# Attention and two feed-forward stages on one core: unread matmuls in front of and among the early heads, and the splitting of x and of most weights moved between engines

## The reference

```python
B, H, S, D = 4, 8, 576, 64                      # batch, heads, positions, width of a head
scores = q @ k.T / sqrt(D);  scores[block_i < block_j] = -1e9      # blocks of 64 positions
attn = exp(scores - max) / (sum + 1e-9);  x = attn @ v             # x: 2304 tokens x 512
h = maximum(maximum(x @ w1, x @ w2), x @ w3)                       # 768 wide
y = h @ w_out                                                      # 512 wide
h2 = y @ w_in;  g = h2 * cos(h2);  out = g @ w_out2                # 2048 wide, back to 512
```

## Time and profile before

| | us |
|---|---|
| median of 3 runs (1001.79 to 1003.62) | 1003.39 |
| the profiled execution, its own time | 1003.43 |
| its span, first to last instruction | 1001.6 |
| PE busy | 967.4 (97%) |
| PEld busy | 874.0 (87%) |
| DVE busy | 579.4 (58%) |
| ACT busy | 572.1 (57%) |
| POOL busy | 188.6 (19%) |

### The profile page before, as it was taken

The page is one execution under the profiler, slowest core; times in us unless marked ns, Lnnn a source line. Parts: engine busy times, 40 slices in busy tenths (PEclk is TensorE's granted clock), DMA queues, the critical chain, the costliest instruction groups (busy, mean ns, idle before and its releaser), DMA issues.

```text
span 1001.6 us, 16447 instructions
## 1 busy us (share of the span) xinstructions
PE 967.4 (97%) x5808; PEld 874.0 (87%) x5808; DVE 579.4 (58%) x1155; ACT 572.1 (57%) x1294; POOL 188.6 (19%) x168
## 2 busy tenths in 40 slices
PE   7998899999999999999999999999999999999998
PEld 6877789889989989999999987789999999999996
DVE  5665566776455655555411257767657566576564
ACT  4576465676455555555322256676656666666665
POOL 2385312322221212212134412210000000000000
PEclk9997799999999999999999999999999999999999
DMA  9242222232222222121051060010010010100000
GB/s 259 60 123 56 61 83 77 79 89 76 71 60 72 60 61 72 49 71 38 19 187 56 1 211 13 1 64 1 1 64 0 0 63 0 63 0 0 31 1 32
DMA packets 58144, 58.16 MB, mean 58 GB/s; under 512 B 26048, under 2 KB 42208, under 8 KB 58080
## 3 DMA queue, kind: packets, MB, share of 16 engines
q1 hardware_dynamic: 55824, 56.73, 18.9%
q10 hardware_dynamic: 2256, 0.59, 0.3%
HBM read 47.78 MB, written 9.52 MB: 57 GB/s over the span
## 4 chain that ended last, share of the span: by engine, by line
PE 73%; DVE 7%; ACT 6%; issue 3%; POOL 1%; ACTq 0%
PE M_ps L670 8%; PE M_ps L672 7%; PE M_ps L671 7%; PE T_ps L625 6%; PE O_ps L643 5%; PE S_ps L743 3%; PE S_ps L536 3%; PE S_ps L742 3%; PE S_ps L741 3%; PE M_ps L680 3%; DVE rest L948 3%; PE M_ps L719 2%; PE O_ps L719 2%; PE M_ps L717 2%; PE O_ps L717 2%
## 5 line engine op out<-in xcount | busy, mean ns | idle before, releaser
L670 PE MATMUL M_ps<-x,w_h 128*128 128x288 f32 (+2 forms) x576 | 178.5, 310 | 0.9 <-POOL w_l L1237 0.9
L672 PE MATMUL M_ps<-x,w_h 128*128 128x288 f32 (+2 forms) x576 | 171.3, 297 | 0.0
L671 PE MATMUL M_ps<-x,w_l 128*128 128x288 f32 (+2 forms) x576 | 171.3, 297 | 0.0
L1185 ACT ACTIVATE away<-rest 128x384 f32<-128x384 f32 x96 | 50.4, 525 | 115.2 <-DVE rest L948 115.2
L670 PEld LDWEIGHTS M_ps<-x,w_h 128*128 128x128 f32 x576 | 109.8, 191 | 3.6 <-issue 1.0
L671 PEld LDWEIGHTS M_ps<-x,w_l 128*128 128x128 f32 x576 | 110.1, 191 | 0.0
L672 PEld LDWEIGHTS M_ps<-x,w_h 128*128 128x128 f32 x576 | 109.9, 191 | 0.0
L849 DVE TENSOR_TENSOR pt_l<-T_ps,pt_h 128x384 fp32r<-128x384 f32 (+2 forms) x120 | 68.9, 574 | 55.1 <-ACT pt_h L1107 55.0
L1091 ACT ACTIVATE prob<-S_ps,neg_max 128x512 f32<-128x512 f32 (+4 forms) x144 | 83.0, 582 | 16.9 <-DVE neg_max L834 16.9
L1107 ACT ACTIVATE pt_h<-T_ps 128x384 fp32r<-128x384 f32 (+2 forms) x120 | 60.6, 505 | 54.3 <-PE T_ps L625 50.7
L625 PE MATMUL T_ps<-ident,prob 128*128 128x128 f32 (+2 forms) x456 | 88.5, 282 | 0.0
(11 more groups left out here) (138 smaller groups left out, 2451.0 us busy)
## 6 DMA issues: line engine op xcount, KB each, us to landing
k_raw<-kT SPq DMA_DIRECT2D x64, 144.0 KB, 2.8
q_raw<-qT SPq DMA_DIRECT2D x48, 144.0 KB, 2.7
y_raw<-y_d SPq DMA_DIRECT2D x6, 768.0 KB, 4.6
out<-o_out SPq DMA_DIRECT2D x18, 256.0 KB, 2.1
v_raw<-v SPq DMA_DIRECT2D x32, 128.0 KB, 2.7
win_raw<-w_in SPq DMA_DIRECT2D x16, 256.0 KB, 6.5
w_raw<-w_out SPq DMA_DIRECT2D x16, 256.0 KB, 5.5
inv_b<-inv_d SPq DMA_DIRECT2D x24, 144.0 KB, 3.1
```

The lines of the kernel that those rows point to most:

```text
L670: mm(o, w_h, x_h, start=k == 0, stop=False)
L671: mm(o, w_l, x_h, start=False, stop=False)
L672: last = mm(o, w_h, x_l, start=False, stop=k == KM - 1)
```

## The change

PE starts with 12 matmuls of 512 columns on a tile of zeros (`WARM`), whose result nobody reads, and from the third early head on puts one more unread matmul of 512 columns in front of each head's scores. The mask of the early heads is added on the 64 rows of the head instead of on all 128. In the main part the high part of x is written by ACT; its low part stays on DVE but stands later in the period. All pieces of w1, w2, w3 and w_out are 512 elements wide; their low parts, and those of w_out2, are made by DVE. POOL keeps those of w_in. Pieces of the first feed-forward stage are split in periods 0 to 6 instead of 0 to 4, at places named W in the orders instead of at the end of the period. `piece`, `early` and `walk` follow this.

```diff
-LAG = {"tA": 1, "tB0": 1, "tB1": 1, "tB2": 1, "vA": 1, "vB": 1, "inv": 1, "inv_out": 1, "inv_in": 1, "take": 1, "norm": 2,
-       "split": -1, "load": -2, "load_v": -1}
+LAG = {"tA": 1, "tB0": 1, "tB1": 1, "tB2": 1, "vA": 1, "vB": 1, "inv": 1, "inv_out": 1, "inv_in": 1, "take": 1,
+       "norm": 2, "norm_low": 2, "split": -1, "load": -2, "load_v": -1}
...
-DVE_PERIOD = ["inv", "sA", "tA", "sC", "tB0", "norm", "G2", "tB1", "sD", "tB2", "split", "G1", "take", "G3"]
-ACT_PERIOD = ["tA", "eA", "tB0", "eC", "G2", "tB1", "split", "tB2", "eD", "G1", "take", "split_v", "G3"]
+DVE_PERIOD = ["inv", "sA", "tA", "sC", "tB0", "norm", "G2", "tB1", "sD", "tB2", "split", "norm_low", "G1", "W1", "take", "W2", "G3"]
+ACT_PERIOD = ["tA", "eA", "tB0", "eC", "G2", "tB1", "norm", "split", "W2", "tB2", "eD", "W1", "G1", "take", "split_v", "G3"]
...
-SP_PERIOD = ["load", "G2", "inv_out", "G1", "inv_in", "load_v", "G3"]
+SP_PERIOD = ["load", "G2", "inv_out", "G1", "inv_in", "load_v", "W1", "G3"]
...
-W_COLS = [(0, P), (P, P), (2 * P, 2 * P), (4 * P, 2 * P)]
-W_OF = [next(n for n, (c0, w) in enumerate(W_COLS) if c0 <= f * P < c0 + w) for f in range(KF1)]
-PIECES = [("w%d" % (j + 1), None, n) for n in range(len(W_COLS)) for j in range(3)]
+PIECES = [("w%d" % (j + 1), None, f * P) for f in range(KF1) for j in range(3)]
...
-PIECES += [("w_out", k, 0) for k in range(0, KF1, 2)]
+PIECES += [("w_out", k, 0) for k in range(KF1)]
...
-W_AHEAD = 12
...
+W_EARLY_HIGH = {4: (0,), 5: (1,), 6: (2,)}
+W_EARLY_LOW = {8: (0, 1), 9: (2,)}
+W_HIGH = {0: (3, 4, 5), 1: (6, 7, 8, 9), 2: (10, 11, 12), 3: (13, 14, 15), 4: (16, 17, 18), 5: (19, 20, 21), 6: (22, 23)}
+W_LOW = W_HIGH
...
+W_AHEAD = 18
...
-        if s[0] == "G":
-            out += ["G"] * ((slots + places - int(s[1:])) // places)
+        if s[0] in "GW":
+            places = sum(o[0] == s[0] for o in names)
+            out += [s[0]] * (((slots if s[0] == "G" else pieces) + places - int(s[1:])) // places)
...
+WARM = 12
...
+            if name == "W":
+                if pieces:
+                    step("weights", pieces.pop(0))
...
+        consts_set, warm_set = sem("consts_set"), sem("warm_set")
+        w_high, w_low, win_low, w2_low = sem("w_high"), sem("w_low"), sem("win_low"), sem("w2_low")
...
-                return (wo_raw[:, k:k + 2, :], wo_h[:, k:k + 2, :], wo_l[:, k:k + 2, :],
-                        w_out[k * P:(k + 2) * P, :].rearrange("(k p) f -> p k f", p=P))
+                return wo_raw[:, k, :], wo_h[:, k, :], wo_l[:, k, :], w_out[k * P:(k + 1) * P, :]
...
                     pe.wait_ge(e_exped, a - 3)
                 half, p = slice(D * (a % 2), D * (a % 2) + D), a // 2
+                if a >= 2:
+                    mm(E_ps[a % 4], mask_l[:], ke_h[:, 0:2, :].rearrange("p a s -> p (a s)"), start=True, stop=True)
                 for t in SCORES["A"]:
                     n, tile = KEYS[t], slice(P * t, P * (t + 1))
                     o = E_ps[a % 4][:, S_AT[t]:S_AT[t] + n]
                     mm(o, qe_h[half, p, tile], ke_h[half, p, 0:n], start=True, stop=False)
                     mm(o, qe_h[half, p, tile], ke_l[half, p, 0:n], start=False, stop=False)
                     mm(o, qe_l[half, p, tile], ke_h[half, p, 0:n], start=False, stop=False)
-                    last = mm(o[:, n - BLOCK:n], mask_l[:], mask_r[:], start=False, stop=True)
+                    last = mm(o[:, n - BLOCK:n], mask_l[half, :], mask_r[half, :], start=False, stop=True)
...
-                        pe.wait_ge(w_low, W_OF[f] * 3 + j + 1)
+                        pe.wait_ge(w_low, f * 3 + j + 1)
...
-                            if c == 0 and k % 2 == 0:
-                                pe.wait_ge(w_low, N_W123 + k // 2 + 1)
+                            if c == 0:
+                                pe.wait_ge(w_low, N_W123 + k + 1)
...
+
+            pe.wait_ge(warm_set, 1)
+            for _ in range(WARM):
+                mm(O_ps[:, 0:BANK], pt_l[:, 0:P], pt_l[:, 0:BANK], start=True, stop=True)
...
-                    pe.wait_ge(w_low, N_IN + f + 1)
+                    pe.wait_ge(w2_low, f + 1)
...
+            def split_weights(p):
+                raw, hi, lo, _ = piece(p)
+                dve.wait_ge(w_high, p + 1)
+                V.tensor_tensor(lo, raw, hi.bitcast(F32), ALU.subtract).then_inc(w_low if p < N_P1 else w2_low, 1)
...
                 V.tensor_tensor(mine, mine, inv_b[:, pair % 2, q0:], ALU.mult).then_inc(x_normed, 1)
-                dve.wait_ge(x_normed, pair + 1)
+
+            def normalise_low(n):
+                q0, b, pair = first_query(n), n // H, n // 2
+                mine = x_f[:, pair % 2, q0:]
                 hi, lo = (x[:, b % 2, part, pair % KM, q0:] for part in range(2))
-                V.tensor_scalar(hi, mine, 1.0, None, ALU.mult).then_inc(x_high, 1)
                 dve.wait_ge(x_high, pair + 1)
                 V.tensor_tensor(lo, mine, hi.bitcast(F32), ALU.subtract).then_inc(x_lowed, 1)
...
+            V.memset(pt_l[:, 0:BANK].bitcast(F32), 0.0).then_inc(warm_set, 1)
...
-            V.memset(mask_l[0:1, 0:BLOCK].bitcast(F32), 1.0).then_inc(consts_set, 1)
-            early(early_step, DVE_EARLY)
-            walk(step, DVE_PERIOD)
+            for row in (0, D):
+                last = V.memset(mask_l[row:row + 1, 0:BLOCK].bitcast(F32), 1.0)
+            last.then_inc(consts_set, 1)
+            early(early_step, DVE_EARLY, W_EARLY_LOW)
+            walk(step, DVE_PERIOD, W_LOW)
...
-            def chunk(c):
+            def chunk(c, split=False):
 
                 last = isinstance(c, int) and c == NC2 - 1
                 for f in range(1, KF2):
                     tile(c, f, last)
+                    if split:
+                        split_weights(N_IN + f)
...
-            chunk(0)
+            split_weights(N_IN)
+            chunk(0, split=True)
...
+            def normalise(n):
+                q0, b, pair = first_query(n), n // H, n // 2
+                act.wait_ge(x_normed, pair + 1)
+                A(x[:, b % 2, 0, pair % KM, q0:], x_f[:, pair % 2, q0:], ACT.Copy).then_inc(x_high, 1)
...
-            early(early_step, ACT_EARLY)
-            walk(step, ACT_PERIOD)
+            early(early_step, ACT_EARLY, W_EARLY_HIGH)
+            walk(step, ACT_PERIOD, W_HIGH)
...
-                sub(lo, raw, hi.bitcast(F32), ALU.subtract).then_inc(w_low, 1)
+                sub(lo, raw, hi.bitcast(F32), ALU.subtract).then_inc(win_low, 1)
...
-                elif name == "weights":
-                    split_weights(a)
...
-            for p in range(N_IN, len(PIECES)):
-                split_weights(p)
```

38 lines of the change are left out of this document (19 added, 19 removed).

## The result

The changed kernel takes 986.96 us (median of 4 runs, 985.13 to 988.22), the kernel before 1003.5 us beside it: ratio 0.9838, 95% interval 0.9818 to 0.9857. It is faster by 16.5 us (1.6%), not by 32.5, and lies outside the range. The profiled executions have spans of 985.7 and 1001.6 us, 15.9 us apart.

What follows compares the result with a forecast made beforehand. PE, with a matmul in flight 97% of the span, was taken as the bound; gains of 6 + 15 + 0.5 + 0.5 + 10.5 = 32.5 us off 1003.43 gave 971 us, own range 966 to 975, 8 times in 10 962 to 982.

Steps and rivals of the forecast that it cites:

- Nobody waits for x until the next batch's groups: Main part: the reason given why ACT can write x's high parts, eight more in each half; no cost set for it.
- the third stretch near 137 us: Main part: third stretch of lowered granted clock (0.71 over 135 to 140 us), left as it is, no gain counted.
- A: Early heads: at full clock DVE sets the pace, 2.74 instead of 3.93 us a head; 6 us gained, bounds 0 and 8.
- 0.5 for the entry: Start of the main part: the clock may be up already, worth up to 1.9 us; 0.5 us taken.
- That it rises I take for likely: Early heads: twelve matmuls back to back likely raise PE's clock; its staying up until the last head was called less sure.
- cost nothing: Start: twelve unread matmuls take 5.1 us at 1.2 GHz, within the 6.5 us for which PE is idle there.
- less what the mask on 64 rows saves: Early heads: unnumbered saving, set against the 2.6 us that six inside unread matmuls cost if the clock is low.
- Rival 1: Early heads: the clock does not rise ahead of them or falls among them; A is 0 or slightly less, 977 us; chance 0.25.
- B: Main part: two long waits ahead of the product with v and the slow clock after them go; 15 us, bounds 8 and 17.
- +0.5: Main part: 1 us of new PE waiting against 1.5 us saved on ACT's and POOL's pieces; net gain 0.5 us, bounds -5 and +3.
- rival 3: Periods 0 to 6: DVE becomes the late one, held by POOL once each period; B pays 10.5 us, 981 us; chance 0.10.
- C: Second stage's first chunk: without POOL's hold a tile takes 4.19 instead of 4.87 us; 10.5 us gained, bounds 6 and 11.

Runs made afterwards that it cites:

- clock-up kernel: Changed kernel with x's low part early, twelve unread matmuls ahead, six ahead of the third early head, three in each head from the third: 970.72 us, 0.9693.

## Why the prediction was wrong, point by point

**"Nobody waits for x until the next batch's groups"** is the step that failed worst. It is true as it stands, and I didn't go on to those groups: the change puts x's low part behind q's split, one step ahead of the first group that reads it. The sum had nothing for it; it gives 10.2 us back, 6.2 us of them as three waits of PE. Moving the step alone recovers 8 to 10 us, and x's move alone shows the same loss (9.8 us) without any other edit. Of the three boundaries the prediction looks at one only ("the third stretch near 137 us"), and for its clock. That stretch gave 1.4 us because the clock happened to stay up behind an unchanged wait: luck, which none of the terms had.

**A, 6 us and 0.5 for the entry.** Measured 1.4 us at head 0's product. "That it rises I take for likely" was right for 3 us: PE waited 1.31 us for q's low part, and the clock fell. I costed the twelve ("cost nothing") and the inner ones rightly for a low clock, 2.6 us against 2.7 to 3.1 measured, and then left "less what the mask on 64 rows saves" without a number. It was the largest term of this part: 5.1 us at head 0's product. The working behind A does hold where the clock stays up: in the clock-up kernel heads are 2.66 us apart (forecast 2.74) and 7.8 us are gained at head 0's product (forecast 6.5). What failed is the assumption that twelve matmuls ahead and one in each head keep it up. Rival 1 stands for this case; it had the clock right and the mask missing.

**B, 15 us.** The mechanism is right: the two waits and the low clock behind them are gone, and x's move alone is worth 14.7 us from head 0 to head 6. "+0.5" for VectorE's pieces had the wrong sign: they cost 2 to 4 us, as PE's waits for probabilities in periods 0 to 4. That is rival 3 in kind (bound -5), though hardly for its reason: GpSimd holds only three of the 21 pieces, by 0.6 us each, behind the first of PE's new waits. Heads 0 to 6 gave 13.0 us in all, where 15 + 0.5 were forecast.

**C, 10.5 us.** Measured 10.3 us in the changed kernel and 10.4 alone, with the clamp and the tile as forecast.

**Sum.** 1.4 + 13.0 + 1.4 - 10.2 + 10.3 = 15.9 us, where 6.5 + 15.5 + 10.5 = 32.5 were forecast: 5.1 us are missing in A, 2.5 in B, 0.2 in C and 10.2 at the boundaries, and 1.4 came by luck.

What stays open: why a wait of the same length lets the clock fall in one execution and not in the next (0.66, 0.50 or 1.00 behind the same 1.22 us, and 970 to 980 us for one kernel), and whether the 0.3 us around the mask is a drain or part of the 128 rows' own product.

## What to carry to other kernels

When a change delays a product, find its first reader in every part of the schedule, in the periods where a new batch begins above all, and read from the trace how long the product lies ready: 4.5 us here, against a step that moved by 6.8. Work made to keep TensorE's clock up has to bridge the waits too, or it is only more work at the low clock: eighteen unread matmuls lost about 2 us here against none, while thirty-six, six of them in the gap, won 4.4 to 4.7. A trace differs from the next by 1.4 us and more wherever the clock may fall behind a wait, so a difference of that size wants the place where it arises, and more than one execution. Where an engine holds another up, shorter pieces at places between the other's can be worth more than moving the work to the engine that waits: 2 to 4 us here.

## What the runs showed of the hardware

A mask product of 64 columns on 128 rows costs 0.3 us more than one on 64 rows where products on 64 rows stand on both sides of it, and 0.51 us for a head with two masks, at the lower clock. A wait of 1.22 us in front of the same scores is followed by a granted clock of 1.00 in some traces (122 to 127 us in the changed kernel) and of 0.66 or 0.50 in others, which costs 1.4 us at 0.66. A GpSimd subtraction in flight holds VectorE's 320-column copy (2.39 instead of 0.33 us) and its subtraction of two SBUF tensors (2.06 instead of 0.49). It works the other way too: with the pieces on VectorE, a GpSimd subtraction that takes 0.87 us alone took

```profile
56.61 2.02 POOL L1290 TENSOR_TENSOR v_s<-v_raw,v_s 128x320 fp32r<-128x320 f32 x1 [3.49 <-ACT v_s L1103]
```

in the run with x wholly on VectorE, where two pieces of VectorE, 1.28 us together, start at the same 56.61 us. In the changed kernel GpSimd starts first in three places, and VectorE's piece takes 1.31 instead of 0.68 us, here in the first of them:

```profile
67.83 0.87 POOL L1296 TENSOR_TENSOR v_s<-v_raw,v_s 128x320 fp32r<-128x320 f32 x1
67.93 1.31 DVE L839 TENSOR_TENSOR w_l<-w_raw,w_h 128x512 fp32r<-128x512 f32 x1
```

By the rule of the Trainium skill that the prediction drew on (SBUF — State Buffer, "Who interferes with whom"), whoever starts first keeps the ports; the trace agrees in both directions.
